# Unit 0 of a fused attention and two-layer kernel in two half-width tiles instead of one full-width tile

## The reference

```python
# gated linear attention: batch 4, 8 heads, 768 tokens, head size 48
f = 1 / (1 + exp(-f_logit))
for t in range(S):
    state = f[:, :, t, :, None] * state + k[:, :, t] (outer) v[:, :, t]
    y[:, :, t] = q[:, :, t] @ state
x = y as (3072 tokens, 384)
# first layer: 384 -> 2048 -> 384
h = x @ w_in
g = where(h >= 1, h, where(h <= -1, 0, (h + 1) ** 2 / 4))
x = g @ w_out
# second layer: 384 -> 1536 -> 384
out = (silu(x @ w_gate) * (x @ w_val)) @ w2_out
```

## Time and profile before

| | us |
|---|---|
| median of 3 runs | 1027.89 |
| lowest and highest | 1027.58, 1028.88 |
| the profiled execution | 1029.0 |
| its span in the profile | 1027.2 |
| TensorE busy | 994.6 (97%) |
| TensorE weight load | 828.3 (81%) |
| VectorE busy | 489.2 (48%) |
| ScalarE busy | 466.1 (45%) |
| GpSimd busy | 427.3 (42%) |
| HBM read, written | 52.89 MB, 9.44 MB |

### The profile page before, as it was taken

The page is one execution under the profiler, slowest core; times in us unless marked ns, Lnnn a source line. Parts: engine busy times, 40 slices in busy tenths (PEclk is TensorE's granted clock), DMA queues, the critical chain, the costliest instruction groups (busy, mean ns, idle before and its releaser), DMA issues.

```text
span 1027.2 us, 19928 instructions
## 1 busy us (share of the span) xinstructions
PE 994.6 (97%) x8277; PEld 828.3 (81%) x8277; DVE 489.2 (48%) x615; ACT 466.1 (45%) x851; POOL 427.3 (42%) x360
## 2 busy tenths in 40 slices
PE   4789999999999999999999999999999999999998
PEld 4668688888888888888888888888888888888886
DVE  7879948745954874584355422222222222232221
ACT  5865667657667765766355322221222222221221
POOL 6759736652763665385265222222222222222222
PEclk9999999999999999999999999999999999999999
DMA  9540133015005201300541010010100100000000
GB/s 353 197 157 2 63 108 151 1 45 184 32 3 173 86 2 51 116 32 2 185 139 47 1 62 1 10 53 1 58 4 1 62 1 1 32 0 1 31 1 32
DMA packets 17802, 63.61 MB, mean 62 GB/s; under 512 B 1968, under 2 KB 2352, under 8 KB 16944
## 3 DMA queue, kind: packets, MB, share of 16 engines
q1 hardware_dynamic: 17712, 62.33, 16.8%
HBM read 52.89 MB, written 9.44 MB: 61 GB/s over the span
## 4 chain that ended last, share of the span: by engine, by line
PE 89%; POOL 4%; issue 2%; DVE 2%; ACT 1%; DMA 1%; SPq 0%; ACTq 0%; POOLq 0%; DVEq 0%
PE acc L568 11%; PE acc L569 10%; PE acc L570 10%; PE bank L595 7%; PE bank L594 7%; PE bank L596 7%; PE hid L554 6%; PE hid L556 6%; PE hid L555 6%; PE bank L407 4%; PE hid L595 2%; PE hid L594 2%; PE hid L596 2%; POOL keys L1117 2%; PE bank L474 2%
## 5 line engine op out<-in xcount | busy, mean ns | idle before, releaser
L1159 POOL TENSOR_TENSOR g_lo<-prod,g_hi 128x512 fp32r<-128x512 f32 x72 | 93.1, 1293 | 347.7 <-ACT g_hi L846 347.7
L1152 POOL TENSOR_TENSOR g_lo<-act_tmp,g_hi 128x512 fp32r<-128x512 f32 x96 | 127.3, 1326 | 166.2 <-ACT g_hi L807 166.2
L1050 DVE TENSOR_TENSOR sig<-sig,bank 128x512 f32<-128x512 f32 x72 | 49.5, 688 | 275.4 <-ACT sig L840 275.4
L846 ACT CAST g_hi<-prod 128x512 fp32r<-128x512 f32 x72 | 44.7, 621 | 248.1 <-PE acc L570 248.1
L1117 POOL TENSOR_TENSOR keys<-keys,gates 128x512 f32<-128x512 f32 x82 | 107.9, 1317 | 73.3 <-PE bank L407 48.3
L554 PE MATMUL hid<-x_hi,win_hi 128*128 128x512 f32 (+1 forms) x291 | 117.0, 402 | 2.8 <-DVE act_tmp L1038 2.4
L568 PE MATMUL acc<-g_hi,wout_hi 128*128 128x512 f32 x288 | 114.2, 397 | 1.2 <-POOL g_lo L1152 1.2
L556 PE MATMUL hid<-x_hi,win_lo 128*128 128x512 f32 (+1 forms) x291 | 113.7, 391 | 0.0
L555 PE MATMUL hid<-x_lo,win_hi 128*128 128x512 f32 (+1 forms) x291 | 113.4, 390 | 0.0
L569 PE MATMUL acc<-g_lo,wout_hi 128*128 128x512 f32 x288 | 112.3, 390 | 0.0
L570 PE MATMUL acc<-g_hi,wout_lo 128*128 128x512 f32 x288 | 112.2, 390 | 0.0
(11 more groups left out here) (102 smaller groups left out, 1932.9 us busy)
## 6 DMA issues: line engine op xcount, KB each, us to landing
gates<-in_f_dram SPq DMA_DIRECT2D x12, 512.0 KB, 5.1
queries<-in_q_dram SPq DMA_DIRECT2D x12, 512.0 KB, 4.9
keys<-in_k_dram SPq DMA_DIRECT2D x12, 512.0 KB, 4.7
values<-in_v_tok_dram SPq DMA_DIRECT2D x6, 1024.0 KB, 7.5
q_tok<-in_q_tok_dram SPq DMA_DIRECT2D x12, 384.0 KB, 7.7
k_tok<-in_k_tok_dram SPq DMA_DIRECT2D x12, 384.0 KB, 8.2
x_dram<-x_out SPq DMA_DIRECT2D x6, 768.0 KB, 3.3
x_raw<-x_dram SPq DMA_DIRECT2D x6, 768.0 KB, 5.5
```

Source lines behind the costliest of these rows:

```text
L1152: pool.tensor_tensor(g_lo[:, c % RING, :], act_tmp[:, 2 + c % 2, :], g_hi[:, c % RING, :].bitcast(F32), ALU.subtract).then_inc(g_lo_done, 1)
```

## The change

Unit 0 goes through the first layer in two *narrow* tiles of 256 columns: tile 0 is batches 0 and 1, tile 1 is batches 2 and 3. The layer has seven tiles now (`TILES = UNITS + 1`): `m` = 0 and 1 are narrow, `m` = 2 to 6 are units 1 to 5 as before.

- Unit 0's attention is done by groups. Group 0 runs ahead of the first chunk (`h` below 0), group 1 within the 16 chunks of tile 0. Unit 1's attention is within tile 1.
- A narrow chunk takes half a buffer: `part(m, c)` picks a half of the ring's two buffers, so four chunks are in flight (`back` = 4). The first product has three banks (`hid` and `acc[2]`, which the narrow tiles don't need, since `acc_of` puts three results of 256 columns in `acc[0]` and `acc[1]`). Second products stand four chunks behind (`NARROW_LAG`); the last two chunks of tile 1 each issue two, so that two are open when the wide tiles begin.
- Ten matmuls of zeros open TensorE's program (`WARM_EARLY`); `keep_warm` stands behind group 0's levels alone.
- The weight splits of the first layer are spread over the half steps of the start and of tile 0 (`W1_HI`, `W1_LO`, `W2_HI`, `W2_LO`): two of eight low parts of `w_in` are split ahead of the first chunk, all eight low parts of `w_out` in tile 0.
- The loads of group 1 and of the weights are issued in another order, gates are loaded earlier, `keys_tok` lies over `q_tok`, and x1 of unit 0 is stored in two halves.

```diff
-LAG = 2
-WARM, WARM_FROM, WARM_LAST = 4, 4, 6
+LAG, NARROW_LAG = 2, 4
+WARM_EARLY, WARM, WARM_LAST = 10, 4, 6
...
-FIRST = Plan(own=(), diag=(18, 20), own_v=(21, 22), place=(), sigmoid=(-6, -5), gated=(-6, -4),
...
+FIRST = Plan(own=(), diag=(-18, 11), own_v=(-14, 14), place=(), sigmoid=(-32, -20), gated=(-32, -12),
...
+             step=by_half((-30, -27, -24, -21, -18), (-8, 1, 4, 7, 10)),
...
+W1_LO = ((-14, -10, -6), (3, 5, 7, 9, 11))
...
+W2_LO = ((), (2, 4, 6, 8, 10, 12, 14, 15))
...
 def turns(m, h):
 
-    now = [(m, h + HS)] if m >= 0 else []
-    if m + 1 < UNITS:
-        now.append((m + 1, h))
-    if m + 2 < UNITS and h - HS >= H_FIRST:
-        now.append((m + 2, h - HS))
+    now = [(m - 1, h + HS)] if m >= 1 else []
+    if 0 <= m < UNITS:
+        now.append((m, h))
+    if m + 1 < UNITS and (m < 0 or h - HS >= H_FIRST):
+        now.append((m + 1, h - HS))
     return now
...
+def back(m):
+
+    return 2 if m > 1 else 4
+
+
+def part(m, c):
+
+    return slice(0, UT) if m > 1 else slice(c // 2 % 2 * UT // 2, (c // 2 % 2 + 1) * UT // 2)
...
+    def hid_of(m, c):
+
+        return hid[c % 2][:, :] if m > 1 else narrow_hid[(m * FC1 + c) % 3][:, 0:UT // 2]
+
+    def acc_of(m, dm):
+
+        return acc[dm][:, :] if m > 1 else acc[dm // 2][:, dm % 2 * UT // 2:(dm % 2 + 1) * UT // 2]
...
-            if n >= 2:
-                pe.wait_ge(activated, n - 1)
...
+            if n >= (2 if m > 1 else 3):
+                pe.wait_ge(activated, n - (1 if m > 1 else 2))
...
+        def projected(m, c):
+
+            n = chunk1(m, c)
+            if m > 1:
+                return (n - LAG,)
+            if m == 1 and c >= FC1 - (NARROW_LAG - LAG):
+                n = chunk1(m, 2 * c - FC1 + NARROW_LAG - LAG)
+                return n - NARROW_LAG, n - NARROW_LAG + 1
+            return (n - NARROW_LAG,) if n >= NARROW_LAG else ()
```

More of the change, by code:

```diff
@@ L317, in store_last, with load_first @@
                 sp.dma_start(out[UNITS - 1][:, dm], result[:, dm, :]).then_inc(stored, 16)
-        for g in range(2):
+        def load_first(g):
             load_f(0, (g,))
@@ L406, in level @@
                 for half in range(2):
-                    last = pe.matmul(of(a, s)[rows(half), x * R:(x + 1) * R],
+                    last = pe.matmul(t[rows(half), x * R:(x + 1) * R],
                                      keys[:, bp, half * HALF:(half + 1) * HALF],
@@ L437, in outputs @@
         def outputs(a, b):
-            i = Y0 + b
-            free(a, i)
+            free(y_fill(a, b))
+            y = bank[y_fill(a, b) % 3]
             if a < PLAIN:
@@ L482, in outputs @@
                     pe.wait_ge(dense_in, 16)
-                last = pe.transpose(of(a, i)[:, DM:DM + P], keys[:, BP - 1], dense[:, :])
+                last = pe.transpose(y[:, DM:DM + P], keys[:, BP - 1], dense[:, :])
             last.then_inc(filled, 1)
         def turn_keys(a, i):
-            free(a, TK0 + i)
+            free(tk_fill(a, i))
             pe.wait_ge(k_scaled, (a + 1) * SCALES)
@@ L491, in turn_keys @@
                 c = x * 2 * D
-                last = pe.transpose(of(a, TK0 + i)[:, c:c + P], keys[:, i * A_BANK + x], dense[:, :])
+                last = pe.transpose(bank[tk_fill(a, i) % 3][:, c:c + P], keys[:, i * A_BANK + x], dense[:, :])
             last.then_inc(filled, 1)
         def key_values(a, g):
-            i = KV0 + g
-            free(a, i)
-            pe.wait_ge(act_took, a * ACT_A_UNIT + ACT_Y + 3 + g)
+            free(kv_fill(a, g))
+            pe.wait_ge(act_took, act_takes(a, (ACT_Y if a else FIRST_ACT_Y) + 3 + g))
             for x in range(BP // 2):
@@ L566, in project @@
                 hi, lo = (t[:, c % 2, dm * P:(dm + 1) * P] for t in w[c // 2][0:2])
-                o = acc[dm][:, :]
-                pe.matmul(o, hi, g_hi[:, c % RING], start=first, stop=False)
-                pe.matmul(o, hi, g_lo[:, c % RING], start=False, stop=False)
-                last = pe.matmul(o, lo, g_hi[:, c % RING], start=False, stop=last_chunk)
+                o = to(dm)
+                pe.matmul(o, hi, g_hi[:, c % RING, p], start=first and dm in starts, stop=False)
+                pe.matmul(o, hi, g_lo[:, c % RING, p], start=False, stop=False)
+                last = pe.matmul(o, lo, g_hi[:, c % RING, p], start=False, stop=last_chunk and dm in stops)
             last.then_inc(out_done, 1)
@@ L618, in _ @@
         pe.wait_ge(cleared, 3)
-        for h in range(H_FIRST, HS):
+        zeros = state_apart[:, :, :].rearrange("p x d -> p (x d)")[:, 0:P]
+        for _ in range(WARM_EARLY):
+            pe.matmul(hid[1][:, 0:P], zeros, zeros, start=True, stop=True)
+        for h in range(HS):
             for a, place in turns(-1, h):
                 attention(a, place)
-        for m in range(UNITS):
+        for m in range(TILES):
             for c in range(FC1):
```

483 lines of the change are left out of this document (265 added, 218 removed).

## The result

| | before | changed |
|---|---|---|
| median, us | 1028.05 (4 runs) | 1038.05 (4 runs) |
| lowest and highest | 1027.58, 1028.88 | 1036.46, 1039.18 |
| the profiled execution, its span | 1029.0, 1027.2 | 1036.46, 1034.7 |

The ratio is 1.0089, with a 95% interval of 1.0077 to 1.0101: the change makes the kernel **about 9 us slower** by the ratio (10.0 by the medians). The forecast was 1023.2, with a range up to 1033. The other 1.6 to 2.5 us they leave open.

The account below looks back on a forecast made before the run. VectorE was taken to pace the stretch from 35.5 us to unit 1's last attention level, TensorE's work the rest: +1.8 us at that level and -6.5 behind it give -4.7, 1027.9 to 1023.2 us; range 1014 to 1033.

Parts of the forecast that it names:

- First narrow product at 35.5: Start of the layer on TensorE: first 256-column product at 35.5 us instead of 57.1, bounds 33 and 39.
- Half-width VectorE operation 0.34 us: VectorE's clamps and maxima on 256 columns: 0.34 us each, from the slope between 512 and 768 columns.
- Rival 3: Each half-width VectorE operation pays more fixed cost: 0.05 us more each gives -2.2 us, 1025.7; chance 0.08.
- VectorE's work from 35.5 us, 85.7: VectorE's work left between 35.5 us and the mark: 108.2 in all less 22.5 already done, 85.7 us.
- the mark: Start of the last level of unit 1's attention on TensorE: 123.64 us before, forecast at 125.4.
- rival 1: Ahead of the mark, VectorE is fed without gaps and GpSimd disturbs it less: about 1017 us; chance 0.20.
- VectorE through at 125.0: VectorE's work ahead of the mark: 85.7 us at its old busy share 0.958 takes 89.5, ending at 125.0.
- The mark 0.4 us behind VectorE's last scaling: Unit 1's last level on TensorE starts at 125.4, 0.4 us after VectorE is through at 125.0.
- Nothing idle behind the mark: TensorE hardly waits behind the mark before, and was assumed not to after the change.
- -6.5 us of owed work: TensorE's unit 0 blocks still open at the mark: 18.1 us instead of 24.6, 6.5 us less.
- Rival 2: VectorE waits near 68 us for the second half's outputs, 5.3 us plus clock 1.5: +2.1, about 1030; chance 0.27.
- TensorE's floor of 113: TensorE's own work from 35.5 us, 75 plus about 2.5 for changes, lets the mark come at about 113 earliest.

## Why the prediction was wrong

The forecast was -4.7 us; the profiled executions differ by +7.5. Step by step:

- **First narrow product at 35.5: right.** It starts at 34.62. The chain worked out from the earlier trace rows held to a microsecond at its end. On the way it was up to 2 us late (the whole blocks at 23.82 for 26.0), and a wait of 1.9 us for ScalarE's last scores, which the chain had as its bound, took most of that back.
- **Half-width VectorE operation 0.34 us: right.** They start 0.33 to 0.34 apart (101.33, 101.67, 102.00), each lasting 0.41 to 0.42. Rival 3, and the estimate of 0.39 by the Trainium skill's VectorE: DVE Perf Modes, "The TRN2 errata", are not borne out as a spacing; as the duration of a single operation the page's figure is near. The page's point, that small tiles pay a fixed part, does hold (0.335 for 256 columns against 0.60 for 512), and it was in the sum.
- **VectorE's work from 35.5 us, 85.7: too high.** It was 80.6. Of the 5.1 us, 1.5 had been done before 35.5 (23.95 us for 22.5). Most of the rest is less disturbance by GpSimd: up to the mark 24 scalings took 21.1 us (24.2 before), and eight weight splits 9.6, for the 10.9 that the sum had (8.0 and three at 0.95). That is rival 1's mechanism, worth 4.4 us; own values took 1.5 more than forecast.
- **VectorE through at 125.0, by its old share of 0.958: this is the step that failed.** It was through at 129.2. With 5.1 us less work than forecast it idled 13.1 us instead of 3.8. Where it idled, these two windows of the changed kernel show (columns as in the earlier trace rows):

```profile
57.40:92.40 35.00, 30.33 (x452) 29.11 (x452) 22.87 (x38) 24.05 (x50) 26.50 (x20) 1.00 0.50 167
92.40:129.18 36.78, 28.75 (x465) 27.09 (x460) 36.11 (x49) 20.98 (x45) 25.80 (x27) 0.95 0.17 55
```

  12.1 of the 13.1 us lie in the first window, **ahead of unit 1's levels**. There VectorE waited 5.1 us for ScalarE's squares, 2.7 for the rounded outputs, 2.2 for a weight half that ScalarE casts, 1.2 for the key-value products and 0.9 for first products. In the second window, with unit 1's levels, it did pace: busy 36.11 of 36.78 us, 0.98. What had gone wrong is when these levels begin. VectorE's first scaling for them, in the kernel before and in the changed one:

```profile
74.51 0.68 DVE L948 TENSOR_TENSOR queries<-queries,gates 128x512 f32<-128x512 f32 x1
...
93.23 2.13 DVE L1055 TENSOR_TENSOR queries<-queries,gates 128x512 f32<-128x512 f32 x2
```

  Before, they begin at half step 6 of unit 0's chunks, in the changed kernel at half step 0 of tile 1, behind all 16 chunks of tile 0: 18.7 us later, though the layer starts 22.5 us earlier. From there to its last scaling ahead of the mark VectorE took 36.0 us, for 41.1 before. The share of 0.958 came from a stretch (60 to 115.6) with unit 1's levels in it from 74.5 on the earlier trace rows; I spread it over one whose first 57 us hold none of them, and whose order I had not followed.
- **Why TensorE idles while VectorE is full.** From the first of these scalings to the last TensorE was busy 39.84 of 41.13 us before and is busy 27.92 of 35.95 now. Two or three half steps lay between two levels before, three lie there now, but a narrow chunk and its second product last 2.15 us for about 4.1. The products that hid VectorE's work are half as long. The prices of the runs (VectorE 0.7 us per us, GpSimd 0.45, part of it through VectorE's lengths, and, for what can be told, ScalarE 0.15) fit VectorE as the pace of this stretch (theory A), with the other hand-overs (theory B) close behind it: half of the takes gone, VectorE itself waits 4.0 us. That the shorter products are why TensorE idles is argued from these windows.
- **The mark 0.4 us behind VectorE's last scaling: wrong by 3.8.** The whole blocks' keys stand in GpSimd's queue behind a g_lo that waited 2.64 us for ScalarE's rounding; they were done at 133.3, and the last level, 0.68 us late for them, ran at 133.40. My check of GpSimd was by its total (61.35 of 80.1), and a total does not show that it ends the chain. Half-length key scalings gave back 3.4 us in all.
- **Nothing idle behind the mark: wrong by 3.4.** From 133.4 to 168.0 TensorE idled 3.8 us, for 0.4 before, the largest wait 2.29 for the last scores (L834), for between the last level and the outputs lie three half steps of narrow products (places 18 and 21, 1.08 us each, 3.2 in all) where two wide ones lay before (21 and 23, 2.05 each, 4.1). Outputs two half steps later gave back 2.6 us. Of the -6.5 us of owed work, 5.7 were there, 1.5 of it behind unit 1's first product; the other 0.8 stays open.
- Sum: (129.2 - 125.0) + 3.8 at the mark, 3.4 + 0.8 behind it, 12.2 together, and -4.7 + 12.2 = +7.5.
- **Rival 2 was the right sign and the wrong place.** The outputs began at 67.75 and ended at 71.0, ahead of its 72.4, and VectorE waited 1.5 and 1.2 us for them, not 5.3. They are two of the waits ahead of unit 1's levels. TensorE's own loss is spread over a dozen waits of 0.7 to 2.3 us.
- **TensorE's floor of 113** was a floor, and nothing near it was reached. That TensorE was dense from 71 to 91 us was not a bound either: 5.4 us less brought 1.2 in one pair of kernels and 0.5 in the other, neither told from none.

What stays open: what sets the pace from 57 to 92 us, where VectorE idled most, for no run took work off ScalarE or GpSimd there; how much of TensorE's saving the clock took; and whether an order exists in which the halves win. The obvious rival is one of place: unit 1's levels begun well within tile 0, where VectorE has 12 us free. They were tried three half steps earlier and no more, which gave 3.2 us, with 9 to regain. That the short chunks cost what they do is argued from the timelines and from the priced work; a variant with the same early start and wide chunks for unit 1's attention was not tried.

## What to carry to other kernels

When a tile is halved so that it can start early, the work that was hidden behind its chunks gets half the cover in each, and may itself begin later than before. Find the engine that is full in the old kernel, and ask at which time its long work can begin in the new order; time in which it idles ahead of that is not made good. An engine's mean busy share of one stretch is no forecast for another order. Count for every hand-over what stands between producer and consumer, in us, before and after. To find out who paces a stretch, leave out some of each engine's work in turn, and compare in the traces how long the other engines' instructions are: here less work on GpSimd also made VectorE's shorter. An engine that is dense for 20 us may be no bound.

## What the runs showed of the hardware

- TensorE's granted clock in a stretch is not fixed by the kernel: two profiles of the changed kernel have 1.00 and 0.95 from 60 to 93.8 us. One place of a fall, in the changed kernel at 110 us, behind waits of 1.62 and 2.12 us with one level of 1.15 us between them:

```profile
105.33 1.15 PE L509 MATMUL bank<-right_q,keys 128*64 128x64 f32 x32 [1.62 <-POOL keys L1224]
108.60 1.69 PE L509 MATMUL bank<-right_q,keys 128*64 128x64 f32 x32 [2.12 <-ACT right_q L799]
110.22 0.58 PE L674 MATMUL acc<-g_hi,wout_hi 128*128 128x256 f32 x1
...
111.02 0.41 PE L674 MATMUL acc<-g_hi,wout_hi 128*128 128x256 f32 x1
...
112.82 0.28 PE L661 MATMUL acc<-x_lo,win_hi 128*128 128x256 f32 x1
```

  There the 256-column matmuls start 0.21 us apart instead of 0.12 (1.2 GHz instead of 2.4), up to 112.3 us.
- A VectorE scaling took 0.69 us with GpSimd idle and 2.31 at 51.64 us, beside a weight split on GpSimd that began at 50.86 and ended at 53.40; it was through at 53.95, about its own length later. By the Trainium skill, SBUF — State Buffer, "SBUF: two separate sides", the two engines share one pair of ports, which the one holds for its whole instruction while the other stands (where VectorE has two SBUF inputs, as here); this pair of instructions agrees. Halving GpSimd's and VectorE's own work together brought the mean of 20 scalings from 0.984 to 0.863 us. With GpSimd's key scalings halved alone, VectorE's 49 instructions from 92.5 to 127.6 us were busy 34.22 us instead of 36.19.
